# Mixer of attention and two MLPs on one core: first MLP product by Strassen's scheme, attention in head pairs

## What is computed

```python
q_n, k_n = rmsnorm(q, g_q), rmsnorm(k, g_k)
scores = q_n @ k_n.transpose(0, 1, 3, 2) / sqrt(64)
attn = exp(scores - max); attn = attn / (sum(attn) + 1e-9)
x = heads_side_by_side(attn @ v)                 # (4, 448, 768)

xn = (x - mean(x)) / sqrt(var(x) + 1e-6) * g_ln  # over the 768
x = x + maximum(xn @ w1a, 0) @ w2a

u = x + (x.transpose(0, 2, 1) @ U @ V).transpose(0, 2, 1)
out = u + maximum(u @ w1b, 0) @ w2b
```

## Time and profile before

| | before |
|---|---|
| median of 3 runs | 1797.57 us |
| lowest, highest | 1797.34, 1797.84 us |
| span of the profiled execution, first to last instruction | 1794.6 us |
| own time of the profiled execution | not listed apart; 2.7 to 3.2 us lie between its span and the runs |
| TensorE matmul, weight load busy | 98%, 92% |
| VectorE, ScalarE, GpSimd busy | 51%, 39%, 11% |
| mean DMA rate | 101 GB/s |

### The profile page before, as it was taken

One profiled execution on the slowest core, in us unless ns is written; L12 is line 12 of the kernel. 1 busy time (PEld: TensorE's weight loads), 2 busy tenths in 40 slices (PEclk: granted clock), 3 DMA queues, 4 the chain that ended last, 5 costly groups with the idle time before them and its releaser, 6 DMA issues.

```text
span 1794.6 us, 29017 instructions
## 1 busy us (share of the span) xinstructions
PE 1766.4 (98%) x10272; PEld 1655.9 (92%) x10272; DVE 913.4 (51%) x1595; ACT 706.3 (39%) x1268; POOL 202.1 (11%) x201
## 2 busy tenths in 40 slices
PE   6999999999999999999999999999999999999998
PEld 5999999899999999999999999999999999999997
DVE  7999999743344444444444444444433433343332
ACT  5777777522333323332333233323222322232221
POOL 6666666000000000000000000000000000000000
PEclk9999999999999999999999999999999999999999
DMA  2222224233333233333333333332433333333320
GB/s 73 69 69 72 68 71 139 87 106 116 113 106 103 93 111 101 106 106 106 105 108 100 102 100 106 106 106 89 138 121 106 97 131 121 106 99 128 121 88 31
DMA packets 205744, 180.41 MB, mean 101 GB/s; under 512 B 12497, under 2 KB 179281, under 8 KB 205649
## 3 DMA queue, kind: packets, MB, share of 16 engines
q1 hardware_dynamic: 203280, 173.51, 30.3%
q10 hardware_dynamic: 2368, 5.51, 0.8%
HBM read 173.48 MB, written 5.51 MB: 100 GB/s over the span
## 4 chain that ended last, share of the span: by engine, by line
PE 80%; DVE 0%; issue 0%; ACT 0%
PE h_ps L733 39%; PE y_ps L750 38%; PE h_ps L680 1%; PE h_ps L669 1%; PE h_ps L698 1%; PE h_ps L706 0%; PE y_ps L658 0%; DVE in_nat L891 0%; ACT in_hi L786 0%; DVE in_lo L854 0%; DVE in_lo L851 0%; DVE y_t L927 0%
## 5 line engine op out<-in xcount | busy, mean ns | idle before, releaser
L844 DVE TENSOR_TENSOR w_lo<-w_raw,w_hi 128x768 fp32r<-128x768 f32 x190 | 182.0, 958 | 674.0 <-ACT w_hi L782 674.0
L750 PE MATMUL y_ps<-h_hi,w_hi 128*128 128x448 f32 x1152 | 424.4, 368 | 0.0
L733 PE MATMUL h_ps<-in_hi,w_hi 128*128 128x448 f32 x1152 | 415.9, 361 | 3.1 <-DVE in_lo L851 1.1
L733 PE MATMUL h_ps<-in_hi,w_lo 128*128 128x448 f32 x1152 | 417.9, 363 | 0.0
L750 PE MATMUL y_ps<-h_hi,w_lo 128*128 128x448 f32 x1152 | 417.8, 363 | 0.0
L750 PE MATMUL y_ps<-h_lo,w_hi 128*128 128x448 f32 x1152 | 417.7, 363 | 0.0
L733 PE MATMUL h_ps<-in_lo,w_hi 128*128 128x448 f32 x1152 | 417.4, 362 | 0.0
L781 ACT ACTIVATE w_hi<-w_raw 128x768 fp32r<-128x768 f32 x189 | 159.7, 845 | 538.1 <-PE y_ps L750 538.1
L817 ACT ACTIVATE h_hi<-h_ps 128x448 fp32r<-128x448 f32 x192 | 104.7, 545 | 380.1 <-PE h_ps L733 338.5
L733 PEld LDWEIGHTS h_ps<-in_hi,w_hi 128*128 128x128 f32 x1152 | 215.6, 187 | 19.1 <-DVE in_lo L851 1.5
L733 PEld LDWEIGHTS h_ps<-in_lo,w_hi 128*128 128x128 f32 x1152 | 216.2, 188 | 15.8
(11 more groups left out here) (90 smaller groups left out, 1407.3 us busy)
## 6 DMA issues: line engine op xcount, KB each, us to landing
w_raw<-in_moe_w_ch SPq DMA_DIRECT2D x384, 384.0 KB, 3.8
qk_raw<-in_q SPq DMA_DIRECT2D x48, 112.0 KB, 2.0
qk_raw<-in_k SPq DMA_DIRECT2D x48, 112.0 KB, 2.1
qt_raw<-in_q_t SPq DMA_DIRECT2D x48, 112.0 KB, 2.5
v_nat<-in_v SPq DMA_DIRECT2D x48, 112.0 KB, 2.0
out<-o_nat ACTq DMA_DIRECT2D x12, 336.0 KB, 5.0
out<-in_nat ACTq DMA_DIRECT2D x4, 336.0 KB, 3.1
u_sb<-in_moe_U SPq DMA_DIRECT2D x4, 56.0 KB, 2.5
```

Of the source, the lines that this page charges most:

```text
L733: last = nc.tensor.matmul(h_ps[j % 2][:, :S], w[:, j % NW, c, :], x[:, c, :], start=(c == 0 and t == 0), stop=(c == DC - 1 and t == 2))
L750: last = nc.tensor.matmul(y_ps[c][:, :S], w[:, j % NW, c * P:(c + 1) * P], x[:, j % 2, :], start=(j == 0 and t == 0), stop=(j == FC - 1 an ...
L844: nc.vector.tensor_tensor(w1_lo[:, r], w1_raw[:, r], w1_hi[:, r].bitcast(F32), ALU.subtract)
```

## The change

The whole kernel is written anew; what it computes is the same. In the lines below, numbers are those of the kernel after.

**First MLP product.** A stage now takes two batches (896 positions), so there are 4 stages. The 768 input rows, the 3072 hidden columns and the 896 positions are each cut in two, and the 2 x 2 blocks are multiplied by Strassen's scheme in Winograd's form: 7 products of half-size operands, P1 to P7, in the place of 8. For a pair of hidden blocks (a "group", 12 per stage) each product is 3 row chunks times 3 terms = 9 matmuls of 448 columns, 63 in all. Four sums of weight blocks (`weight_sum`, L996, 128 x 384) are made on VectorE for each group. Four sums of the input per chunk and stage (`make_sums`) are made on GpSimd, once a stage. The results are put together on VectorE (`combine`, L1027 to L1039, five additions of 128 x 448) after a ScalarE copy of P1.

**Second product.** Plain: after each two groups, 12 products M of 12 matmuls (two batches, two chunks, three terms), two to an output pair of banks, which VectorE adds into the SBUF array `acc` (`gather`, L1050).

**Order of the MLP.** One list `prods`: per stage six times (7 products of group 2j, 7 of group 2j + 1, 12 of M). Every engine walks through it; a weight's high part is made four products ahead, its low part three ahead, in a ring of 8.

**Attention.** Two heads make a pair t, 24 pairs; a step n is one tile of 112 query rows of both heads, 96 steps. Scores are now three matmuls per head over 64 rows, head 0 on partitions 0 to 63, head 1 on 64 to 127, into two banks. One maximum covers both heads (112 x 2 x 448). The turned copies, k's scaling and the squares are per pair. Attention's output is turned at once into columns (`turn_x`), twice: as it is, and after the layer normalisation, and goes through DRAM (`xres`, `xnrm`) where it isn't kept.

**The rest.** Products with U and V run as 12 items of two chunks in stages 1 and 2 (`mixing`). Weights lie in DRAM in the order of use; a transfer brings 768 KB for one group or half an M. All loops are written out. The output leaves in the layout (batch, chunk, 128, 448).

The core of the diff:

```diff
@@ TensorE, scores
-                    lhs = q_st[:, slot, i * TP:(i + 1) * TP]
-                    nc.tensor.matmul(scores[i][:TP, :S], lhs, k_hi[:, slot, :], start=True, stop=False)
-                    nc.tensor.matmul(scores[i][:TP, :S], lhs, k_lo[:, slot, :], start=False,
-                                     stop=True).then_inc(scores_done, 1)
+                    for a, b in ((q_hi, k_hi), (q_hi, k_lo), (q_lo, k_hi)):
+                        for h in range(2):
+                            rows = slice(h * D, (h + 1) * D)
+                            last = nc.tensor.matmul(mm_ps[:TP, 2 * (n % 2) + h, :S], a[rows, t % 2, i * TP:(i + 1) * TP],
+                                                    b[rows, t % 2], start=a is q_hi and b is k_hi, stop=a is q_lo)
@@ TensorE, MLP
-                        last = nc.tensor.matmul(h_ps[j % 2][:, :S], w[:, j % NW, c, :], x[:, c, :],
-                                                start=(c == 0 and t == 0), stop=(c == DC - 1 and t == 2))
+                def product(q):
+                    kind, s, n, k = prods[q]
+                    pe.wait_ge(wlo_done, q + 1)
...
+                        for c in range(HC):
...
+                            for p, (a, x) in enumerate(((0, in_hi), (0, in_lo), (1, in_hi))):
+                                last = nc.tensor.matmul(bank(q), w[a][:, c * P:(c + 1) * P], x[:, k, c],
+                                                        start=k not in ONTO and c == 0 and p == 0,
+                                                        stop=c == HC - 1 and p == 2, skip_group_check=k in ONTO)
@@ VectorE, MLP
-                nc.vector.tensor_tensor(w1_lo[:, r], w1_raw[:, r], w1_hi[:, r].bitcast(F32), ALU.subtract)
-                nc.vector.tensor_tensor(w2_lo[:, r], w2_raw[:, r], w2_hi[:, r].bitcast(F32),
-                                        ALU.subtract).then_inc(w_lo_done, 1)
+                    if k == P5:
...
+                        out, in0, in1, op = w_s1[:], a21, a22, ALU.add
...
+                    nc.vector.tensor_tensor(out, in0, in1, op).then_inc(sum_done, 1)
...
+                    nc.vector.tensor_tensor(w_lo[:, q % RING, :w], weights(q), w_hi[:, q % RING, :w].bitcast(F32),
+                                            ALU.subtract).then_inc(wlo_done, 1)
...
+                    if k == P3:
+                        nc.vector.tensor_tensor(t_c12, bank(q), t_u2, ALU.add).then_inc(comb_done, 1)
...
+                    for b in range(2):
+                        nc.vector.tensor_tensor(acc[:, b, d], bank(q, b), acc[:, b, d], ALU.add).then_inc(ev_done, 1)
@@ SyncE, loads
-            sp.dma_start(w1_raw[:, r], w1_v[ds(g, 1), r].rearrange("a p c f -> (a p) c f")).then_inc(w_in[r], 16)
-            sp.dma_start(w2_raw[:, r], w2_v[ds(g, 1), r].rearrange("a p n -> (a p) n")).then_inc(w_in[r], 16)
+                    if r >= 2:
+                        sp.wait_ge(wlo_done, runs[r - 2][-1] + 1)
...
+                    sp.dma_start(w_raw[r % 2][:].rearrange("p a c -> p (a c)"), src).then_inc(w_in[r % 2], 16)
```

1679 lines of the change are left out of this document (931 added, 748 removed).

## The result

The changed kernel takes 1842.32 us (median of 4 runs, 1819.78 to 1865.37), the kernel before 1797.46 (1797.34 to 1797.84) beside it. The ratio is **1.015 [1.0123, 1.0177]**: slower by 1.5%, and by 2.5% in the medians, where 6.7% less was forecast. The profiled execution is the one of 1865.37 us (span 1863.6, mean granted clock 0.937). The ratios here leave out executions that lie over 1.5% above the fastest of their kernel, and so favour those that lost little clock; the medians don't.

A forecast was written before the change was run, and what follows sets the result against it. It took TensorE, busy 98%, as the bound: its instructions times their spacing. Attention's end at 330, MLP matmuls 1298, side work 29, end 5 and waits 12 make 1674 us, plus 3 outside the span 1677; range 1654 to 1742.

The forecast's parts named there:

- The clock: Sign of being wrong: a granted clock under 0.95 in a stage; no time was put on it.
- If one is late, the turn of exponentials or the next pair's scores are late: Attention: a late helper engine delays these TensorE products; VectorE is nearest to being late; no time given.
- What hides the rest, per pair: Attention: per pair of 13 us, VectorE has 10.5 us of work, ScalarE 9.8 and GpSimd 9.2, all under TensorE.
- Attention's step: Attention: a pair of heads takes 12.98 us on TensorE, a step 3.25 us; 94 steps make 305.5 us.
- The heads do share the array: Attention scores: against the forecast's sharing, the rival had each half-row matmul cost its own 0.2003 us, +58 us, 1735; chance 0.18.
- Going over to the 64-row form and back: Attention: changing matmul form each step costs 0.2 us, 0.8 per pair, between bounds of 0.08 and 0.32.
- MLP matmuls: MLP stages: 6480 matmuls in place of 6912, at 0.2003 us each 1298.0 us, 86.5 us less.
- Waits, 12 us allowed: First input sums and three stage changes: 12 us together, bounds 0 and 30; low parts and loads cost nothing.
- the rival that VectorE bounds the first product: First MLP product: VectorE's 20 instructions per group exceed TensorE's 12.6 us, +52 us, 1729; chance 0.07, slow end 0.04.
- Side work in the MLPs: MLP stages: TensorE's turning of inputs and products with U and V take some 29 us, 27 us less.
- Start and end: First score at 15.5 us, two steps to fill 5 us; after the MLPs an end of 5 us.

The follow-up runs named there:

- e15: The change with second moments buffer, one-column products of maxima and roots, shared normalisation, ScalarE squares, moved second-batch turns, earlier first-group weight sums: 1756.4 us, ratio 0.9774.
- e1: The change with a second buffer for the moments, variances and inverse roots: 1816.3 us, ratio 1.0065.
- e9: The change with a second buffer of the moments and one-column products of maxima and roots: 1794.5 us, ratio 0.9944.
- e10: e9 with the first group's weight sums moved from attention steps 58 to 62 to steps 47 to 51: 1806.4 us.
- e11: e10 with an artificial TensorE stall (two small loads) behind the scores of attention step 20: 1869.4 us, ratio 1.0285.
- e12: e9 with two of the four instructions of each pair's normalisation moved from GpSimd to VectorE: 1794.4 us, ratio 0.994.
- e14: e10 with an artificial TensorE stall (two small loads) ahead of product 200 in the second MLP stage: 1779.0 us, ratio 0.9904.

## Why the prediction was wrong, point by point

- **The clock** was named only as a sign of being wrong ("a granted clock under 0.95 in a stage"), with no price. This is the step that failed: "If one is late, the turn of exponentials or the next pair's scores are late" was left without any price, of the wait or of what follows it. A wait of 3.37 us was followed by 184 us at 0.50, some 80 us. In all, the record has 227 us at 0.50 in attention, some 99 us lost; 470 less 99 is 371, close to e15's 368, which was measured. The four waits over 0.5 us in attention are 7.6 us of these 371. But even at full clock the forecast would have been missed: e15, which makes the same products, took 1756 us, and the range ended at 1742. The terms below are that part, and the step of attention is the largest.
- **What hides the rest, per pair.** VectorE 10.5 and GpSimd 9.2 us of 13 were sums of durations, and nearly right as such, GpSimd's by chance: the power takes 2.94 us, not 3.9, and a pair's normalisation 3.15, not 1.2, since "its rate of 2 ns a column" doesn't hold for four instructions of 128 columns, 0.79 us each. What the sums can't show is order. The aggregation waits for a normalisation of the same step on another engine; two turns meet in one step; one engine holds up the other. I priced no wait in attention except its first fill.
- **Attention's step.** At full clock steps take 3.24 without a turn, 3.62 with k's, 3.88 with x's, 3.92 with the normalised one. My 3.25 was a mean that held 2.75 small records of turning, 0.25 us. The timeline:

```profile
99.91 0.46 PE L619 MATMUL mm_ps<-k_hi,q_hi 64*112 64x448 f32 x2
100.21 0.36 PE L619 MATMUL mm_ps<-k_lo,q_hi 64*112 64x448 f32 x2
100.41 0.37 PE L619 MATMUL mm_ps<-k_hi,q_lo 64*112 64x448 f32 x2
100.71 1.00 PE L639 MATMUL mm_ps<-v,e_t 112*112 112x64 f32 x8
101.54 0.55 PE L627 MATMUL sc_ps<-ident,e_nat 112*112 112x112 f32 x4
101.92 0.91 PE L639 MATMUL mm_ps<-v,e_t 112*112 112x64 f32 x8
102.67 0.55 PE L627 MATMUL sc_ps<-ident,e_nat 112*112 112x112 f32 x4
103.15 0.46 PE L619 MATMUL mm_ps<-k_hi,q_hi 64*112 64x448 f32 x2
```

  **The heads do share the array**: each pair of scores costs 0.20 us, so that rival falls, and the Trainium skill (TensorE: Matmul & The Clock Gate, Packing small matmuls), named there, is borne out: matmuls on other row groups run at once. The six scores hold 0.80 us of the step, as forecast. But the products around them pay too: the eight with v behind them take 0.83 us where the later eight take 0.75, and the last four turns 0.48 where the first four take 0.38. Going over to the 64-row form and back costs nearer 0.4 us than my 0.2, above my upper bound of 0.32. With 0.3 us of idle time at x's and the normalised turns a pair takes 13.98 us, and 14.66 with a normalised turn, for 12.98 forecast. Over 94 steps this is some 35 us.
- **MLP matmuls**: the count is right (6480). Their spacing isn't the 0.2003 of the earlier trace rows. Two pieces of the chain of waits:

```profile
586.53 25.54 PE mm_ps L672 x126
...
1662.25 29.76 PE mm_ps L682 x144
```

  These are 0.2027 and 0.2067 us each. Over the four stages, spacings under 0.215 us come to 24 us more than at 0.2003. The kernel before has 0.200 in each of its stages, so this comes with the change. What sets it stays open: the last stage ran at 0.207 in the traces of the change, e1, e9, e10, e11, e12 and e14, and at 0.203 in the other ten.
- **Waits, 12 us allowed**: gaps inside the products come to 24 us, of them 19 in stages 2 and 3. At their changes VectorE is the bound, as a stretch up to the third stage shows (24.10 of 25 us; before it had 9.91 in a stage):

```profile
1137.00:1162.00 25.00, 22.14 (x108) 19.83 (x107) 24.10 (x35) 14.21 (x31) 14.35 (x12) 1.00 0.43 153
```

  New inputs' low parts, gathering and weights come together there. This is the right form of the rival that VectorE bounds the first product: for some 25 us at each of three changes, not over 48 groups.
- **Side work in the MLPs**: 29 forecast, some 43 measured, from the time between a side product and the MLP products around it. Of the 14 us more, 9.7 are 16 waits of TensorE for xs_lo ahead of the products with U (L694), which the prediction doesn't name.
- **Start and end**: first score at 14.3 (15.5 forecast), the end 4.5 (5).

The sum by its own steps: 1677, plus 35 (attention's step), 8 (its waits), 24 (spacing), 12 (waits in the MLPs) and 14 (side work), less 2 (start and end) is 1768, where the estimate for the profiled execution at full clock is 1766. The clock makes the rest.
